# A dense layer's last products and an expert layer's first ones: reordering the passage between them

## What is computed

```python
h = x @ w_in                                  # dense, 2304 x 2048
g = h * (1.0 / (1.0 + np.exp(-1.702 * h)))
x = g @ w_out                                 # 2304 x 512
logits = x @ w_gate                           # 2304 x 8
expert_idx = np.argmax(logits, axis=1)
...                                           # gate_w: softmax at expert_idx
for e in range(E):
    mask = expert_idx == e
    h = np.maximum(x[mask] @ w1[e], 0.0)      # 1024 wide
    out[mask] = gate_w[mask, None] * (h @ w2[e])
```

## Time and profile before

| | us |
|---|---|
| median of 3 runs (808.04 to 808.32) | 808.28 |
| the profiled execution: its own time | 808.37 |
| the profiled execution: its span | 806.3 |
| PE busy | 776.8 (96%) |
| PEld busy | 711.9 (88%) |
| DVE busy | 361.1 (45%) |
| ACT busy | 307.6 (38%) |
| POOL busy | 322.1 (40%) |
| PE's share of the chain that ended last | 83% |

### The profile page before, as it was taken

The page is one execution under the profiler, slowest core; times in us unless marked ns, Lnnn a source line. Parts: engine busy times, 40 slices in busy tenths (PEclk is TensorE's granted clock), DMA queues, the critical chain, the costliest instruction groups (busy, mean ns, idle before and its releaser), DMA issues.

```text
span 806.3 us, 15801 instructions
## 1 busy us (share of the span) xinstructions
PE 776.8 (96%) x5514; PEld 711.9 (88%) x5515; DVE 361.1 (45%) x908; ACT 307.6 (38%) x714; POOL 322.1 (40%) x280
## 2 busy tenths in 40 slices
PE   7999989999999999999999999999999999999995
PEld 6777777889899989988989998997999999999994
DVE  5777777511224424433443445766763322331321
ACT  3777776633232232232233223253214324425320
POOL 5777776135322222212222223234026716627521
PEclk9999999999999999999999999999999999999998
DMA  8776674011050020010002001051062541621011
GB/s 298 288 253 229 240 267 158 1 53 53 1 183 0 1 78 0 0 49 29 0 0 78 0 0 40 21 199 33 28 221 77 162 144 47 216 72 39 29 59 31
DMA packets 25444, 74.17 MB, mean 92 GB/s; under 512 B 3120, under 2 KB 3632, under 8 KB 25280
## 3 DMA queue, kind: packets, MB, share of 16 engines
q1 hardware_dynamic: 22144, 63.68, 22.6%
q0 software_dynamic: 3264, 10.03, 4.1%
HBM read 61.11 MB, written 12.58 MB: 91 GB/s over the span
## 4 chain that ended last, share of the span: by engine, by line
PE 83%; ACT 4%; POOL 4%; issue 4%; DVE 3%; DMA 1%; SPq 0%; POOLq 0%; ACTq 0%; DVEq 0%
PE pj L701 25%; PE nm L883 16%; PE pj L1301 8%; PE kv L883 8%; PE kv L1317 6%; PE nm L1317 6%; PE nm L1301 5%; POOL sqt L205 2%; POOL sqt L201 2%; ACT feat L417 1%; PE pj L255 1%; PE pj L1330 1%; PE kv L273 1%; PE tr L1288 1%; ACT qfT L397 1%
## 5 line engine op out<-in xcount | busy, mean ns | idle before, releaser
L857 POOL TENSOR_TENSOR gl<-g,gh 128x384 fp32r<-128x384 f32 x96 | 99.2, 1036 | 306.6 <-ACT gh L719 306.6
L714 DVE TENSOR_TENSOR g<-pj,sg 128x384 f32<-128x384 f32 x96 | 53.5, 557 | 220.1 <-ACT sg L709 219.8
L709 ACT ACTIVATE sg<-pj 128x384 f32<-128x384 f32 x96 | 47.2, 492 | 254.1 <-PE pj L701 254.1
L701 PE MATMUL pj<-xh,win_h 128*128 128x384 f32 x384 | 129.5, 337 | 1.2 <-DVE xl L736 1.2
L701 PE MATMUL pj<-xh,win_l 128*128 128x384 f32 x384 | 129.4, 337 | 0.0
L701 PE MATMUL pj<-xl,win_h 128*128 128x384 f32 x384 | 128.9, 336 | 0.0
L701 PEld LDWEIGHTS pj<-xh,win_h 128*128 128x128 f32 x384 | 72.1, 188 | 5.2 <-DVE xl L736 1.5
L701 PEld LDWEIGHTS pj<-xl,win_h 128*128 128x128 f32 x384 | 72.1, 188 | 3.6
L701 PEld LDWEIGHTS pj<-xh,win_l 128*128 128x128 f32 x384 | 72.0, 188 | 0.0
L1301 PE MATMUL pj<-xTh,W 128*128 128x288 f32 x320 | 71.6, 303 | 0.0
L825 DVE SCALAR_TENSOR_TENSOR raw<-tr,xT 128x512 f32<-128x512 f32 x90 | 58.6, 688 | 8.2 <-DVE g L714 7.6
(11 more groups left out here) (255 smaller groups left out, 1695.4 us busy)
## 6 DMA issues: line engine op xcount, KB each, us to landing
wraw<-in_moe_w SPq DMA_DIRECT2D x7, 2048.0 KB, 10.9
ve<-in_v_z SPq DMA_DIRECT2D x16, 585.0 KB, 3.8
qk<-in_qk_n SPq DMA_DIRECT2D x16, 576.0 KB, 5.0
qkT<-in_qk_t SPq DMA_DIRECT2D x15, 576.0 KB, 5.4
y_rows<-ys SPq DMA_DIRECT2D x18, 256.0 KB, 2.3
stage<-in_moe_w_in SPq DMA_DIRECT2D x8, 512.0 KB, 6.2
y_early<-ys SPq DMA_DIRECT2D x12, 256.0 KB, 2.7
stage<-in_moe_w_out SPq DMA_DIRECT2D x4, 512.0 KB, 6.6
```

The source lines that it names most:

```text
L701: mm = eng.matmul(ph[f % 3][:, 0:BT], w[f // F1A][:, c, f % F1A, :], x[:, c, :], start=(c == 0 and w is win_h and x is xh), stop=(c == DC ...
L709: eng.activation(sg[f % 2][:, :], ph[f % 3][:, 0:BT], ACT.Sigmoid, scale=1.702).then_inc(a_sg, 1)
L714: eng.tensor_tensor(g32[f % 2][:, :], ph[f % 3][:, 0:BT], sg[f % 2][:, :], ALU.mult).then_inc(v_g, 1)
L857: eng.tensor_tensor(gl[f % 3][:, :], g32[f % 2][:, :], gh[f % 3][:, :].bitcast(F32), ALU.subtract).then_inc(g_gl, 1)
```

## The change

1. DVE: at slices 14 and 15 of the last block `low_x` comes first, and then only one chunk of w2's low half. POOL makes the other two chunks at the start of its `late`.
2. PE: the 12 routing products alternate with the 12 products of slice 0 of tile 0's `up` (`first_up`), so `up` begins at slice 1 (`made` = 1).
3. Tile 0's low halves `hTl` go from DVE to POOL: ACT makes, besides the high half, a full-precision Relu into one of two places in `yTs`, and POOL subtracts (new L1208). PE now waits for ACT's second pass (`a_hf`) before it writes a bank again; only `down` waits for the subtraction (`h_lo`, before `v_h`).
4. PE: `ranks` moves from behind slice 0 to the middle of slice 2.
5. PE: `down` of tile 0 waits for all of w2's low half at once; `enter` moves forward from the middle of column 3 to the end of column 2, ahead of `turn_x` of piece 1 (before, it stood behind piece 2).

```diff
         def route(k):
             eng.wait_ge(v_yt, k + 1)
             for c in range(DC):
                 mm = eng.matmul(pl[:, k * E:(k + 1) * E], yT[:, k, c, :], wg[:, c, :], start=(c == 0), stop=(c == DC - 1))
-            mm.then_inc(p_l, 1)
+                if c == DC - 1:
+                    mm.then_inc(p_l, 1)
+                beside["first_up"](eng, DC * k + c)
...
         turn(1)
+        eng.wait_ge(v_g, F1 * BLOCKS)
         route(0)
...
@@ gpsimd @@
         def late(eng):
+            for c in range(2, CHUNKS):
+                low(eng, 0, 1, c)
+            for j in range(F2):
+                eng.wait_ge(a_hf, j + 1)
+                eng.tensor_tensor(hTl[:, j, :], yTs[:, j % 2, :], hTh[:, j, :].bitcast(F32), ALU.subtract).then_inc(h_lo, 1)
             eng.wait_ge(y_done, 16 * NT)
             gather(eng, 1)
...
+        def first_up(eng, i):
+            c, a = i // 3, i % 3
+            if a == 0:
+                eng.wait_ge(lo[0], c + 1)
+                eng.wait_ge(v_tx, c + 1)
+            mm = up_one(eng, 0, c, *((HI, xTh), (HI, xTl), (LO, xTh))[a])
+            if i == 3 * DC - 1:
+                mm.then_inc(p_hh, 1)
+
-        def up(eng, t, k, after):
-            for j in range(F2):
-                need(eng, v_h, F2 * t + j - 2)
+        def up(eng, t, k, after, made=0):
+            for j in range(made, F2):
+                if made:
+                    need(eng, a_hf, j - 2)
+                else:
+                    need(eng, h_lo, F2 * t + j - 2)
...
-            up(eng, 0, 0, {0: lambda: ranks(eng, False), F2 - 1: lambda: inverse(eng, 2, PR_INV, V_TILE, V_GATE)})
-            down(eng, 0, 0, {(2, 0): lambda: turn_x(eng, 1, 0), (2, 1): lambda: turn_x(eng, 1, 1),
-                                (3, 0): lambda: (turn_x(eng, 1, 2), enter()), (3, 1): lambda: turn_x(eng, 1, 3)})
+            up(eng, 0, 0, {(2, 1): lambda: ranks(eng, False), F2 - 1: lambda: inverse(eng, 2, PR_INV, V_TILE, V_GATE)}, 1)
+            down(eng, 0, 0, {(2, 0): lambda: turn_x(eng, 1, 0), (2, 1): lambda: (enter(), turn_x(eng, 1, 1)),
+                                (3, 0): lambda: turn_x(eng, 1, 2), (3, 1): lambda: turn_x(eng, 1, 3)})
...
@@ scalar @@
         def late(eng):
             for j in range(F2):
                 high_h(eng, 0, j)
+                need(eng, h_lo, j - 1)
+                eng.activation(yTs[:, j % 2, :], ph[j % 3][:, 0:TOK], ACT.Relu).then_inc(a_hf, 1)
                 if j == 3:
...
@@ vector @@
-            if 14 <= f < 16:
-                low(eng, 0, 1, 2 * (f - 14))
-                low(eng, 0, 1, 2 * (f - 14) + 1)
             if f >= F1 - 2:
                 low_x(eng, 0, f - F1 + 2)
+            if 14 <= f < 16:
+                low(eng, 0, 1, f - 14)
...
-            low_h(eng, 0, 0)
...
-            low_h(eng, 0, 1)
```

More of the change, by code:

```diff
@@ L1061, in experts_part @@
     a_h = sem("a_h")
-    v_h = sem("v_h")
+    h_lo = sem("h_lo")
+    a_hf = sem("a_hf")
     p_yy = sem("p_yy")
@@ L1289, in turn_x, with up_one @@
             mm.then_inc(p_tx, 1)
-        def up(eng, t, k, after):
-            for j in range(F2):
-                need(eng, v_h, F2 * t + j - 2)
+        def up_one(eng, j, c, w, x):
+            return eng.matmul(ph[j % 3][:, 0:TOK], weights(w[0], c * FF2 + j * P), x[:, c, :],
+                              start=(c == 0 and w is HI and x is xTh), stop=(c == DC - 1 and w is LO))
+        def first_up(eng, i):
[12 more added lines that the diff above has]
+                    need(eng, h_lo, F2 * t + j - 2)
                 for c in range(DC):
@@ L1300, in up @@
                     for w, x in ((HI, xTh), (HI, xTl), (LO, xTh)):
-                        mm = eng.matmul(ph[j % 3][:, 0:TOK], weights(w[0], c * FF2 + j * P), x[:, c, :],
-                                        start=(c == 0 and w is HI and x is xTh), stop=(c == DC - 1 and w is LO))
+                        mm = up_one(eng, j, c, w, x)
+                    if (j, c) in after:
+                        after[j, c]()
                 mm.then_inc(p_hh, 1)
@@ L1312, in down @@
                     if d == 0:
-                        if f * D % WCH == 0:
+                        if isinstance(k, int):
+                            need(eng, lo[1], CHUNKS if f == 0 else 0)
+                        elif f * D % WCH == 0:
                             eng.wait_ge(lo[1], CHUNKS * k + f * D // WCH + 1)
-                        eng.wait_ge(v_h, F2 * t + f + 1)
+                        eng.wait_ge(h_lo, F2 * t + f + 1)
                     for w, h in ((HI, hTh), (HI, hTl), (LO, hTh)):
@@ L1392, in late @@
                 ending(last)
-        return ahead, late
+        return ahead, late, first_up
     def scalar():
@@ L1519, in low_h @@
             eng.scalar_tensor_tensor(out=hTl[:, j, :], in0=ph[j % 3][:, 0:TOK], scalar=0.0, in1=hTh[:, j, :].bitcast(F32),
-                                     op0=ALU.max, op1=ALU.subtract).then_inc(v_h, 1)
+                                     op0=ALU.max, op1=ALU.subtract).then_inc(h_lo, 1)
         def rows(eng, t, table, at):
@@ L1672, in late @@
             link(eng, eng.tensor_tensor(start[:, :], end[:, :], nt[:, :], ALU.subtract))
-            low_h(eng, 0, 2)
             link(eng, eng.tensor_scalar(first_sub[:, :], start[:, :], float(SUBS), None, ALU.mult))
@@ L1678, in late @@
             link(eng, eng.tensor_tensor(til[:, :], til[:, :], q[:, :], ALU.add))
-            low_h(eng, 0, 3)
             link(eng, eng.tensor_tensor(sel_t[:, :, :], over(til[:, :], TC), along(io_t[:, :], NT), ALU.is_equal))
-            low_h(eng, 0, 4)
             select(eng, T_L)
-            low_h(eng, 0, 5)
             spread(V_TILE, V_GATE).then_inc(v_val, 1)
-            low_h(eng, 0, 6)
-            low_h(eng, 0, 7)
             eng.wait_ge(p_iv, 2)
@@ L1767, in build @@
                                ((b2, nm0, b0), tr, (nm1, kv), b1, b3), dense)
-        ahead.update((name, first) for name, (first, _) in experts.items())
-        late = {name: last for name, (_, last) in experts.items()}
+        ahead.update((name, parts[0]) for name, parts in experts.items())
+        ahead["first_up"] = experts["tensor"][2]
+        late = {name: parts[1] for name, parts in experts.items()}
         block = ctx.enter_context(nc.Block())
```

## The result

| us | before | after |
|---|---|---|
| median of 8 runs each | 808.20 (807.25 to 809.08) | 806.00 (805.23 to 806.42) |
| the profiled execution: its own time | 808.37 | 805.85 |
| the profiled execution: its span | 806.3 | 803.9 |
| PE busy | 776.8 | 775.5 |
| DVE busy | 361.1 | 354.2 |

The ratio of after to before is 0.9975, with a 95% interval of 0.9966 to 0.9985: 2.0 us faster. The interval is 0.8 us to either side, more than several terms of the sum, so the terms are read from the traces and from experiments.

What follows compares the result with a forecast made beforehand. PE, busy 96% of the span, was taken as the bound. Terms 1.70 + 1.65 - 0.2 - 1.65 + 0.65 + 0.1 made 2.25 us, so 806.0 us from a median of 808.28; 8-in-10 range 804.0 to 808.2.

Steps and rivals of the forecast that it cites:

- part 2: Routing products alternating with slice 0's: the stretch falls from 6.15 to 4.5 us at 2.4 GHz, a gain of 1.65 us.
- the table read: Reads moved ahead of piece 2's turn in `down` overlap 12 products without a wait: gain 0.6 to 0.7 us.
- Part 1: `low_x` ahead of w2's chunks on DVE: `half` of slice 15 starts at 559.43 instead of 561.13, gain 1.70 us.
- the small products alone (3.3 us of them) brought 1.2 GHz: Premise read from the earlier profile: small routing products lowered PE's granted clock to 0.51 in 568.3 to 571.2 us.
- The wait ahead of `inverse`: POOL's subtractions hold DVE's planning chain, so PE waits 1.65 us ahead of `inverse` and 0.2 ahead of `ranks`.
- slice 2's holds `slot`, slice 3's holds `start`: In DVE's planning chain, POOL's subtractions for these slices were to hold these instructions 0.6 us each.
- `ranks` at full clock: On PE, `ranks` no longer meets the low clock: gain 0.1 us.
- Small operations are not held: Rival: POOL holds up no small DVE planning instructions, so no wait at `ranks` or `inverse`: 804.1 us, 10%.
- Whole instructions are held: Rival: DVE and POOL exclude each other for whole instructions, wait at `inverse` 3.4 us: 807.8 us, 10%.
- The clock stays out: Rival: PE's clock falls despite pairing routing products with slice 0's, which ends 1.35 us later: 807.3 us, 13%.
- Pairs cost 0.42 us: Rival: each routing product paired with a slice 0 product takes 0.42 us instead of 0.333: 807.1 us, 3%.
- Slower: Rival: a 3.4 us wait at `inverse` also lowers the clock for `down`'s next 12 to 14 products: 809.3 us, 9%.

Runs made afterwards that it cites:

- experiment 8: The change with POOL's eight subtractions replaced by fills with zeros that read nothing: 803.92 us (one run).
- experiment 5: The change with tile 0's low halves made on DVE from PSUM again, without ACT's second pass and POOL's subtractions: 805.50 us, ratio to before 0.9972.
- experiment 2: The change with the 12 routing products ahead of slice 0's 12 again instead of alternating: 806.05 us, ratio to before 0.9985.
- experiment 9: The change with each of POOL's eight subtractions made twice, same values: 809.04 us (one run).
- experiment 10: The change with `inverse` moved into column 0 of `down`, `ranks` earlier, tile 1's turns and table read later: 805.39 us, ratio to before 0.9971.

## Why the prediction was right, and where it was not

The time came out at the forecast, 806.0. Part of this is luck: the terms that were off have opposite signs (part 2 gained 0.3 us less by the traces, the table read 0.35 more), and the account of the clock behind part 2 is wrong. Term by term:

- **Part 1, 1.70 forecast, 1.67 in the pair of traces and in the trace of the undo, 1.2 to 1.5 in time by the ratios.** Right, with the mechanism: POOL's `gl` of slice 15 was late next (it ended at 559.80, `half` began at 559.85), and the two chunks on POOL cost nothing.
- **Part 2, 1.65 forecast, 1.39 in the pair of traces.** Right for this pair, wrong in its reason. The failed step is "the small products alone (3.3 us of them) brought 1.2 GHz": with the same products together behind a busy PE the clock stayed at 1.00 in three traces. A pair took 0.357 us, not 0.333, which is 0.3 us on twelve and takes back what the pairs save by not waiting for `yT` (1.84 us against 8 x 0.20 = 1.58): apart or in pairs, the stretch is 4.81 or 4.72 us. What part 2 gains is the clock, and part 1 seems to win that too. Against the kernel before that was timed with each, the change gained 2.2 and 1.7 us in median and the version with routing apart 1.8 and 1.2; by the ratios (0.9985 and 0.9986 against 0.9975 and 0.9979) undoing part 2 costs 0.6 to 0.8 us. The intervals overlap.
- **The wait ahead of `inverse`, 1.65 forecast, 1.36 measured; 0.2 at `ranks` forecast, 0.07 of idle time measured.** Right in mechanism. By starts the two together are 1.74 us (13.11 against the 11.37 of experiment 8), since the recorded end of a product lies behind its pace. Of the held instructions, `oh`, `sel_s` and `spread` were named; "slice 2's holds `slot`, slice 3's holds `start`" was off by one instruction each time: `thr` and `first_sub` were held, for 0.50 and 0.56 us against 0.6. `slot` and `start` were ahead of the subtractions by 0.01 and 0.10 us, and the sum does not feel which small instruction is hit. What the step left out is the comparison with the low halves on DVE once parts 1 and 2 are made: PE then waits 0.8 us (experiment 5), so of the 1.36 us only some 0.5 are the move's. The rest comes from where the chain begins: `tot` began 1.05 us behind slice 0's end before (572.30 and 571.25) and 2.67 us behind it in experiment 5 (571.08 and 568.41), because the logits now come with the last pair and `ranks` stands in the middle of slice 2, while the chain itself took 10.4 and 9.8 us. Routing apart with `ranks` early in slice 1 was not tried. By the 2.12 us that DVE stands idle in experiment 2 the chain could begin up to about 2 us sooner there (an estimate), which is more than this wait.
- **The table read, 0.65 forecast, 1.00 measured.** The gap of 0.76 went, as argued. Mis-sized: the 12 products behind the gap took 1.85 us, 0.23 more than those without a gap in front; I had counted the recorded gap alone and bounded the gain by it.
- **`ranks` at full clock, 0.1 forecast, 0.07 measured** (0.16 us by starts before, 0.09 after). Left out of the sum was slice 1, which had paid 0.26 us at the low clock too.

**The rivals.** "Small operations are not held": refuted by `thr` and `first_sub`. "Whole instructions are held": the wait of 3.4 us did not come; DVE is let go 0.14 us before POOL's recorded end, as the earlier trace rows had it (the profile's spans on POOL are rough, so this is a distance between records). "The clock stays out": seen at the routing products in none of nine traces with pairs. "Pairs cost 0.42 us": they took 0.357. "Slower": its mechanism is real, as experiment 9 shows with a wait of 2.6 us; with the wait of 1.4 us the clock stayed at 1.00, in each trace that has it.

**What stays open.** Of 22 runs with the routing products apart, 12 took over 806.5 us (up to 808.3); of 19 of the change, one did. None of those 12 has a trace. Whether the clock fell at the small products in them, or what else cost up to 2 us, is not settled, and so neither is what the pairs are worth, between nothing and 0.8 us.

## What to carry to other kernels

When work is taken off an engine in order to shorten its chain, look at what the receiving engine reads: here one subtraction on GpSimd held back two-operand work on VectorE, and a small instruction of a dependent chain, of 0.2 us, then took 0.7. A wait that a change creates can be bypassed by moving its consumer behind work that is ready: in experiment 10 the wait of 1.4 us went for two of 0.7 together, and the ratio fell by 0.0004 to 0.0008, which is within the intervals. The trace of an undo can show a better version than the change: in experiment 2 DVE stood idle for 2.12 us ahead of the very chain that PE waits for later. And a clock that is low behind some work may be due to that work and to what preceded it, together: an undo of each alone, profiled more than once, helps to tell which.

## What had not been expected of the hardware

- `first_sub`, a TENSOR_SCALAR with one SBUF input of 8 elements, was held as two-input instructions are: 0.73 us beside a POOL subtraction, 0.17 beside a fill. The Trainium skill (SBUF — State Buffer, Who interferes with whom) counts `tensor_scalar` among the operations that can take the shared pair of ports, under conditions on its operands; this row agrees, and `act`, of the same kind, was held to 0.40 us in experiment 9.
- The granted clock fell in 2 of 2 traces of the kernel before, but not at the same product: from slice 0's first on in one, about 1.1 us later in the other.
- Two register reads from a table cost PE 0.94 us where nothing ready stands in front of them, and nothing where 12 products do.
